# A third Q/K buffer, loads moved behind the row transfers, and half of the row transfers issued by ACT, in a fused token mixer

## The chip, the cores and the metric

One core of one Trainium2 chip runs the whole program. The metric is the device time of one execution in microseconds (us); lower is better. Time before: median 774.71 us of 3 runs.

## The reference, cut to what matters

The input has batch 4, 8 heads, 768 tokens and head size 48 (so 384 features). Three stages follow one another.

```python
# 1: recurrence per head, S complex [48, 48]; a = (a_re, a_im) scaled to |a| <= 0.999
for t in range(S):
    S_re, S_im = ar * S_re - ai * S_im + k_t v_t^T, ar * S_im + ai * S_re
    y[t] = q_t @ S_re
# 2: x from y, heads side by side: [4, 768, 384]
h = x.transpose(0, 2, 1) @ U @ V          # rank 32 over the tokens
u = x + h.transpose(0, 2, 1)
x = u + relu(u @ w_ch1) @ w_ch2           # 384 -> 1536 -> 384
# 3
theta = x @ w_theta
y = w_tok_r @ (x * cos(theta)) + w_tok_i @ (x * sin(theta))
u = x + y
out = u + relu(u @ w_ch)
```

## The kernel before

The recurrence is computed as chunked linear attention, six chunks of 128 tokens per batch element ("batch" below, b = 0 to 3; chunks c = 0 to 5). The complex decay is turned into real exponents and phases, so that Q and K of a chunk are multiplied by a decay factor and then by a cosine and by a sine of the phase. The cosine part is r = 0, the sine part is r = 1. Stages 2 and 3 are large fp32 matmuls. Each engine runs its own program, written out by hand, in which everything of one engine stands in a fixed order and all ordering between engines is by semaphores. There is no scheduler.

What happens for chunk c+2 and chunk c of the attention, with the names used below:

- SP issues the load of Q and K (`load_qk`, L330) into one of two buffers `qk_in`, which are parts of the big tile `stream`; 384 KB. The load of chunk c waits until chunk c-2 has been multiplied (`s_Q`).
- ACT computes the decay factors of chunk c+2 (`decays`, L682, six ACTIVATEs L691/L692) for b >= 1. For b = 0 they are ready before the loop.
- DVE multiplies Q and K in place by the factors (`scaled`, L1041) and then writes the cosine product and the sine product (`turned`, L1055), each of which raises `s_Q` by one.
- SP copies the two products into `rows` with a different layout, features of a head on the partitions (`to_rows`, L343). Each part is two DMAs, 256 KB (L357) and 128 KB (L358), so four DMAs per chunk. SP waits for `s_Q` before each part.
- PE transposes K of the product (`key_columns`, L1343), ACT copies that out (`keys_to_sbuf`, L710/L711, four ACTIVATEs), PE computes scores from `rows` (`scores`, 16 matmuls, 96x128), then keys times values (`keys_values`, 16 matmuls 128x96), then the outputs (`values`, 128x128 and 96x128), and transposes the state (`turn_state`, L1375).
- ACT copies keys times values (L735) and the chunk's output (L742, the output copy). DVE masks the scores (L1072) and updates the state (L1089, L1091).

ACT's order within a chunk c is: `keys_to_sbuf(c)`, `decays(c+2)`, `rows_of_x(c-1)` (L718), the copy L735, the output copy L742. In batch 0 two weight pieces are rounded after that (`round_piece`, L867). SP's order for c from 1 is: load of Q/K of chunk c+3, load of V of chunk c+2, rows of chunk c+2. `first_rows` (L651) already issues one pair of row DMAs from ACT, once, at the start of the program.

The two quoted lines that set the waits of a row transfer and of a Q/K load:

```python
sp.wait_ge(s_Q.sem, s_Q.at(b, c) + r + 1)      # L355, in front of each part
sp.wait_ge(s_Q.sem, s_Q.at(b, c - 1))          # L333, the load into a used buffer
```

Of the kernel before, what the change touches and what calls it, by code (L numbers as in the profile page):

```python
# [11 lines left out]
P = 128  # L12
# [17 lines left out]
def token_mixer_program(nc, v, qk_rows, a_rows, U, V, w1, w2, w_tc, w_tok, out):  # L30
# [18 lines left out]
    with ExitStack() as ctx:  # L49
# [42 lines left out]
        a_in = stream[:, 0:2 * A_BUFS * D].rearrange("p (i j d) -> p i j d", i=A_BUFS, j=2)  # L92
        qk_in = [stream[:, at * D:(at + 2) * D].rearrange("p (i j t) -> p i j t", i=G, j=2) for at in (0, 2)]
        tok = nc.alloc_sbuf_tensor_at("tok", [P, 4, 2, S], F32R, offset=stream_at)
# [119 lines left out]
        s_a_in = [sem(f"s_a_in{i}", 2 if i + A_BUFS < C else 1, 16) for i in range(A_BUFS)]  # L214
        s_qk_in = [sem(f"s_qk_in{i}", C // 2, 16) for i in range(2)]
        s_v_in = [sem(f"s_v_in{i}", C // 3, 16) for i in range(3)]
# [106 lines left out]
        def _(sp):  # L323
# [6 lines left out]
            def load_qk(b, c):  # L330

                if c >= 2:
                    sp.wait_ge(s_Q.sem, s_Q.at(b, c - 1))  # L333
                sp.dma_start(qk_in[c % 2], qk_rows[b, c * P:(c + 1) * P, :].rearrange("p (i j t) -> p i j t", i=G, j=2))\
                    .then_inc(s_qk_in[c % 2].sem, 16)

# [6 lines left out]
            def to_rows(b, c):  # L343

                if c >= 3:
                    sp.wait_ge(s_yt.sem, s_yt.at(b, c - 2))
                elif b and c == 2:
                    sp.wait_ge(s_ch.sem, s_ch.at(b - 1, 2 * KD))
                elif b and c == 1:
                    sp.wait_ge(s_mix.sem, s_mix.at(b - 1, 2 * C))  # L350
                elif b:
                    sp.wait_ge(s_mix.sem, s_mix.at(b - 1, 2 * C - 2))
                to = rows[c % 3]
                for r in range(2 if b or c else 1):
                    sp.wait_ge(s_Q.sem, s_Q.at(b, c) + r + 1)  # L355
                    wide, fine = row(r)
                    sp.dma_start(to[wide, :, :, :], QKz[c % 2][:, r, 0:2, :, :]).then_inc(s_rows_in[c % 3].sem, 16)  # L357
                    sp.dma_start(to[fine, :, :, :], QKz[c % 2][:, r, 2, :, :]).then_inc(s_rows_in[c % 3].sem, 16)  # L358
# [42 lines left out]
            def batch(b, last):  # L401
                b_next = b + 1
                for c in range(C - 1):
                    if c + 3 < C and (c >= 1 or b == 0):
                        load_qk(b, c + 3)
                    if c >= 1 and c + 2 < C:
                        load_v(b, c + 2)
                    if c + 2 < C:
                        to_rows(b, c + 2)
                    if b and c == 0:  # L410
                        sp.wait_ge(s_stored[2 * KD - 1].sem, s_stored[2 * KD - 1].at(b, 0))
                        load_v(b, 2)
                    if b and c == 1:
                        store(b - 1, KD)
                        store(b - 1, KD + 1)
# [9 lines left out]
                if not last:  # L425
                    load_a_last(b_next)
                    sp.wait_ge(s_tan.sem, s_tan.at(b_next, C))
                    sp.wait_ge(s_quot.sem, s_quot.at(b_next, C))
                load_tok(b, 0)
                load_tok(b, 1)  # L430
# [7 lines left out]
                if not last:  # L438
                    sp.wait_ge(s_mix.sem, s_mix.at(b, 2 * C - 3))
                    load_qk(b_next, 0)  # L440
                    load_qk(b_next, 1)
                    gains_to_rows(b_next)
                    to_rows(b_next, 0)
                    load_qk(b_next, 2)
                    sp.wait_ge(s_mix.sem, s_mix.at(b, 2 * C))
                    load_v(b_next, 0)
                    load_v(b_next, 1)
# [10 lines left out]
            for c in range(C):  # L458
                load_a(0, c)
            load_qk(0, 0)  # L460
            load_qk(0, 1)
            for i in range(3):
# [9 lines left out]
            to_rows(0, 0)  # L472
            load_qk(0, 2)
            to_rows(0, 1)
            gains_to_rows(0)
            for n in range(2 * PIECES, STAGED):
# [113 lines left out]
        def _(act):  # L590
# [51 lines left out]
            def first_sin_cos(c):  # L642
# [6 lines left out]
                a.activation(sin, sin, ACT.Sin, scale=SIN_TURN).then_inc(s_phasor.sem, 1)  # L649

            def first_rows():  # L651

# [69 lines left out]
            def attention(b, c):  # L722
# [17 lines left out]
                if c >= 1:  # L740
                    act.wait_ge(s_y.sem, s_y.at(b, c))
                a.activation(YT[:, :, :], heads(bank[3][:, :]), ACT.Copy).then_inc(s_yt_sb.sem, 1)  # L742

            def hidden(b, n):
# [144 lines left out]
        def _(dve):  # L889
# [144 lines left out]
            def scaled(b, c):  # L1034

                dve.wait_ge(s_qk_in[c % 2].sem, s_qk_in[c % 2].at(b, c // 2 + 1))
                dve.wait_ge(s_exp.sem, s_exp.at(b, c + 1))
                both, factor = qk_in[c % 2], scale[:, c % 2, :, :, :]
                if b == 0:
# [3 lines left out]
            def turned(b, c, r):  # L1043
# [9 lines left out]
                elif b:  # L1053
                    dve.wait_ge(s_mix.sem, s_mix.at(b - 1, 2 * C - 2))
                d.tensor_tensor(QKz[c % 2][:, r, :, :, :], qk_in[c % 2],  # L1055
                                by.unsqueeze(2).broadcast_to([P, G, 2, P]), ALU.mult).then_inc(s_Q.sem, 1)
# [611 lines left out]
```

## Time and profile before

| | |
|---|---|
| median of 3 runs | 774.71 us (773.43 to 777.81) |
| the profiled execution | 773.47 us |
| its span | 771.7 us |
| mean granted TensorE clock | 0.989 |
| busy: PE, DVE, ACT, POOL | 731.8 (95%), 499.9, 403.8, 223.6 us |
| DMA | 73.48 MB, mean 95 GB/s |
| attention of batch 0, 1, 2, 3 (us from the start) | 48 to 96, 237 to 275, 414 to 453, 592 to 630 |

The span is what the profiler recorded between the first and the last instruction of the program; the execution's own time is 1.8 us longer. Busy times are sums over one engine. In a timeline row the first number is the start and the second how long it lasted, both in us; "x16" is how many instructions it merges. A number in square brackets ("idle before") is the time in which the engine did nothing ahead of that instruction, with what ended it.

### The profile page before, as it was taken

What the parts mean: (1) busy time and instruction counts of PE and PEld (TensorE: products, weight loads), DVE (VectorE), ACT (ScalarE), POOL (GpSimd) and SP (SyncE); (2) the same over time, 40 slices, a digit from 0 to 9 for tenths busy, and PEclk for the clock granted to TensorE, in tenths of its full rate; (3) what the DMA queues carried; (4) which work ended last, traced back from release to release, by engine and by line L of the source; (5) the groups of instructions that cost most, each with busy time, mean ns of one, the idle gap of its engine ahead of it and who ended that gap; (6) DMA issues with size and microseconds to landing.
All of it is one profiled execution on the core that took longest, in us unless ns stands there. A gap on an engine that the chain in (4) does not pass through costs nothing.

```text
span 771.7 us, 13433 instructions
## 1 busy us (share of the span) xinstructions
PE 731.8 (95%) x5118; PEld 704.2 (91%) x5118; DVE 499.9 (65%) x905; ACT 403.8 (52%) x875; POOL 223.6 (29%) x175
## 2 busy tenths in 40 slices
PE   3588999999999999999999999999999999999998
PEld 3578799999999879999999879999999979999998
DVE  7759488798468657696558758597448832224534
ACT  7847456755365447664464537574464621223531
POOL 0006663533520063323430053232530010113350
PEclk9889999999999999999999999999999999999999
DMA  9566620100257750010246860010136940000121
GB/s 301 169 184 180 196 87 1 41 1 2 82 145 213 209 174 1 4 39 1 62 133 184 218 205 21 2 42 1 50 96 185 254 135 23 2 1 0 42 62 62
DMA packets 42735, 73.48 MB, mean 95 GB/s; under 512 B 8784, under 2 KB 23376, under 8 KB 42672
## 3 DMA queue, kind: packets, MB, share of 16 engines
q1 hardware_dynamic: 42384, 72.23, 31.9%
q8 instruction: 41, 0.67, 0.4%
q10 hardware_dynamic: 288, 0.39, 0.2%
q14 instruction: 22, 0.18, 0.1%
HBM read 48.96 MB, written 4.72 MB: 70 GB/s over the span
## 4 chain that ended last, share of the span: by engine, by line
PE 81%; DVE 7%; ACT 4%; DMA 4%; issue 2%; SPq 1%; DVEq 0%; ACTq 0%
PE bank L1302 78%; DMA stream<-stream 2%; DMA region<-stream 1%; PE bank L1507 1%; DVE stream L1041 1%; DVE logr L915 1%; DVE logr L911 1%; PE bank L1418 1%; PE bank L1343 1%; PE bank L1375 1%; SPq L357 1%; DVE phasor L904 1%; DVE stream L1055 0%; SPq L358 0%; DVE ST L1072 0%
## 5 line engine op out<-in xcount | busy, mean ns | idle before, releaser
L1302 PE MATMUL bank<-uT,w_sb 128*128 128x384 f32 x864 | 166.5, 339 | 0.0
L1302 PE MATMUL bank<-hT,w_sb 128*128 128x384 f32 x864 | 165.0, 336 | 0.0
L1302 PE MATMUL bank<-tok,z 128*128 128x384 f32 x864 | 158.7, 337 | 0.6 <-issue 0.2
L1302 PEld LDWEIGHTS bank<-uT,w_sb 128*128 128x128 f32 x864 | 151.6, 190 | 1.8 <-ACT uT L756 1.2
L1302 PEld LDWEIGHTS bank<-hT,w_sb 128*128 128x128 f32 x864 | 151.1, 188 | 0.3 <-DVE hT L1200 0.3
L1302 PEld LDWEIGHTS bank<-tok,z 128*128 128x128 f32 x864 | 149.3, 188 | 1.7 <-POOL tok L539 1.7
L1200 DVE SCALAR_TENSOR_TENSOR hT<-bank,hT 128x384 fp32r<-128x384 f32 x96 | 52.8, 550 | 68.1 <-ACT hT L748 67.7
L748 ACT ACTIVATE hT<-bank 128x384 fp32r<-128x384 f32 x96 | 46.4, 484 | 75.4 <-PE bank L1302 75.3
L539 POOL TENSOR_TENSOR tok<-tok_low,tok 128x768 fp32r<-128x768 f32 x20 | 38.2, 1909 | 86.7 <-ACT tok L778 86.7
L547 POOL TENSOR_TENSOR x_sb<-uT 128x384 f32<-128x384 f32 x24 | 25.1, 1077 | 104.1 <-DVE uT L1194 71.1
L514 POOL TENSOR_TENSOR logr<-stream 128x384 f32<-128x384 f32 x18 | 15.1, 841 | 102.1 <-DMA stream<-in_a 102.1
L534 POOL TENSOR_TENSOR w_sb<-w_raw,w_sb 128x768 fp32r<-128x768 f32 x12 | 26.1, 2189 | 63.7 <-ACT w_sb L867 63.7
L553 POOL TENSOR_TENSOR xs<-x_sb,xs 128x384 fp32r<-128x384 f32 x24 | 27.7, 1173 | 54.5 <-ACT xs L765 54.5
L1302 PE MATMUL bank<-tc_sb,xs 128*128 128x384 f32 x216 | 41.4, 335 | 0.0
L1072 DVE TENSOR_TENSOR ST<-bank,tri 128x512 f32<-128x512 f32 x48 | 32.5, 687 | 13.2 <-PE bank L1302 12.9
L1302 PE MATMUL bank<-xs,tc_sb 128*128 128x384 f32 x216 | 38.9, 337 | 0.0
L519 POOL TENSOR_TENSOR phasor<-stream,phasor 128x384 f32<-128x384 f32 x18 | 18.8, 1046 | 68.6 <-ACT phasor L665 68.6
L1302 PEld LDWEIGHTS bank<-tc_sb,xs 128*128 128x128 f32 x216 | 37.9, 188 | 0.0
L1302 PEld LDWEIGHTS bank<-xs,tc_sb 128*128 128x128 f32 x216 | 37.4, 188 | 0.0
L539 POOL TENSOR_TENSOR tok<-scale,tok 128x768 fp32r<-128x768 f32 x16 | 29.4, 1848 | 25.9 <-ACT tok L778 25.9
L1302 PE MATMUL bank<-region 96*128 96x128 f32 x256 | 33.3, 286 | 3.6 <-DMA region<-stream 3.6
L1302 PEld LDWEIGHTS bank<-region 96*128 96x128 f32 x256 | 31.7, 200 | 4.1 <-DMA region<-stream 4.0
(183 smaller groups left out, 1309.5 us busy)
## 6 DMA issues: line engine op xcount, KB each, us to landing
stream<-in_qk SPq DMA_DIRECT2D x24, 384.0 KB, 3.9
tok_low<-in_w_tok SPq DMA_DIRECT2D x20, 384.0 KB, 3.5
stream<-in_a SPq DMA_DIRECT2D x19, 384.0 KB, 3.8
scale<-in_w_tok SPq DMA_DIRECT2D x16, 384.0 KB, 4.2
w_raw<-in_w SPq DMA_DIRECT2D x12, 384.0 KB, 7.8
region<-qk SPq DMA_DIRECT2D x16, 256.0 KB, 3.6
region<-stream SPq DMA_DIRECT2D x15, 256.0 KB, 3.2
stream<-in_v SPq DMA_DIRECT2D x16, 192.0 KB, 4.3
```

The costliest lines, as they stand in the source:

```text
L357: sp.dma_start(to[wide, :, :, :], QKz[c % 2][:, r, 0:2, :, :]).then_inc(s_rows_in[c % 3].sem, 16)
L514: ins = g.tensor_tensor(to, part, part, ALU.mult)
L519: g.tensor_tensor(phasor[:, c, 1, :], a_part(b, c, 1), phasor[:, c, 1, :], ALU.mult)\
L534: g.tensor_tensor(part[1], raw, part[0].bitcast(F32), ALU.subtract).then_inc(s_split.sem, 1)
L539: g.tensor_tensor(tok[:, m % 4, 1, :], tok_raw(m)[1], tok[:, m % 4, 0, :].bitcast(F32), ALU.subtract)\
L547: g.tensor_tensor(x_sb[:, n, :], uT[:, 0, kd, :].bitcast(F32), uT[:, 1, kd, :].bitcast(F32), ALU.add)\
L553: g.tensor_tensor(xs[0][:, 1, n % KD, :], x_sb[:, n, :], xs[0][:, 0, n % KD, :].bitcast(F32), ALU.subtract)\
L748: a.activation(hT[:, n % 3, 0, :], hidden_bank[n % 3][:, 0:N2], ACT.Relu).then_inc(s_hid_hi.sem, 1)
L904: d.tensor_tensor(mag, mag, qk[:, c * D:(c + 1) * D], ALU.add).then_inc(s_den.sem, 1)
L1072: d.tensor_tensor(ST[:, 4 * i:4 * i + 4, :], heads(score_bank[i][:, :]), tri[:, :].unsqueeze(1).broadcast_to([P, 4, P]), ALU.mult)\
L1200: d.scalar_tensor_tensor(hT[:, n % 3, 1, :], hidden_bank[n % 3][:, 0:N2], 0.0, hT[:, n % 3, 0, :].bitcast(F32), ALU.max, ALU.subtract)\
L1302: return t.matmul(o, lhsT, rhs, start=start, stop=stop, is_transpose=turned)
```

## The change

A tile `qk_third` is added and Q/K loads go round over three buffers. The load of chunk c waits for chunk c-3. SP puts the rows of chunk c+2 in front of the Q/K load of chunk c+4 and of the V load of chunk c+2. The load of chunk 2 for the next batch goes to an earlier place, in front of the first token-weight load; in batch 0 it goes to the program's start. From the third chunk on SP issues only the cosine part of the rows. The sine part is issued by ACT (`sine_rows`), directly behind the output copy of chunk c, for chunk c+2.

```diff
-        qk_in = [stream[:, at * D:(at + 2) * D].rearrange("p (i j t) -> p i j t", i=G, j=2) for at in (0, 2)]
+        qk_third = sb("qk_third", [P, 2 * D])
+        qk_in = [at.rearrange("p (i j t) -> p i j t", i=G, j=2)
+                 for at in (stream[:, 0:2 * D], stream[:, 2 * D:4 * D], qk_third[:, :])]
...
-                if c >= 2:
-                    sp.wait_ge(s_Q.sem, s_Q.at(b, c - 1))
-                sp.dma_start(qk_in[c % 2], ...)
+                if c >= 3:
+                    sp.wait_ge(s_Q.sem, s_Q.at(b, c - 2))
+                sp.dma_start(qk_in[c % 3], ...)
...
-                for r in range(2 if b or c else 1):
+                for r in range(2 if c < 2 and (b or c) else 1):
...
                 for c in range(C - 1):
-                    if c + 3 < C and (c >= 1 or b == 0):
-                        load_qk(b, c + 3)
+                    if c + 2 < C:
+                        to_rows(b, c + 2)
+                    if c + 4 < C:
+                        load_qk(b, c + 4)
                     if c >= 1 and c + 2 < C:
                         load_v(b, c + 2)
-                    if c + 2 < C:
-                        to_rows(b, c + 2)
...
                     sp.wait_ge(s_quot.sem, s_quot.at(b_next, C))
+                    load_qk(b_next, 2)
                 load_tok(b, 0)
...
                     to_rows(b_next, 0)
-                    load_qk(b_next, 2)
...
-            load_qk(0, 0)
-            load_qk(0, 1)
+            for c in range(3):
+                load_qk(0, c)
...
             to_rows(0, 0)
-            load_qk(0, 2)
             to_rows(0, 1)
+            load_qk(0, 3)
             gains_to_rows(0)
...
+            def sine_rows(b, c):
+
+                if c >= 3:
+                    act.wait_ge(s_yt.sem, s_yt.at(b, c - 2))
+                elif b:
+                    act.wait_ge(s_ch.sem, s_ch.at(b - 1, 2 * KD))
+                act.wait_ge(s_Q.sem, s_Q.at(b, c + 1))
+                wide, fine = row(1)
+                act.dma_start(rows[c % 3][wide, :, :, :], QKz[c % 2][:, 1, 0:2, :, :]).then_inc(s_rows_in[c % 3].sem, 16)
+                act.dma_start(rows[c % 3][fine, :, :, :], QKz[c % 2][:, 1, 2, :, :]).then_inc(s_rows_in[c % 3].sem, 16)
...
                 a.activation(YT[:, :, :], heads(bank[3][:, :]), ACT.Copy).then_inc(s_yt_sb.sem, 1)
+                if c + 2 < C:
+                    sine_rows(b, c + 2)
...
-                both, factor = qk_in[c % 2], scale[:, c % 2, :, :, :]
+                both, factor = qk_in[c % 3], scale[:, c % 2, :, :, :]
```

ACT's program in a batch from the second on, at chunk 1, before. `region<-bank` L742 is the output copy, `qk<-bank` is `keys_to_sbuf`, `scale<-` are the decay factors, `x_sb<-bank` is `rows_of_x`, `tA<-bank` the copy of keys times values:

```order
L735 ACTIVATE tA<-bank 112x384 [waits s_kv_t,s_kv]
L742 ACTIVATE region<-bank 128x512 [waits s_y,s_yt]
L710 ACTIVATE qk<-bank 128x256 [waits s_kv,s_ktr]
L711 ACTIVATE qk<-bank 128x128
L710 ACTIVATE qk<-bank 128x256 [waits s_kv,s_ktr]
L711 ACTIVATE qk<-bank 128x128
L691 ACTIVATE scale<-logr,minus_mid 128x128 [waits s_qf,s_mid,s_logr]
L692 ACTIVATE scale<-logr,marks 128x128
```

The same place of ACT's program in the changed kernel:

```order
L748 ACTIVATE tA<-bank 112x384 [waits s_kv_t,s_kv]
L755 ACTIVATE region<-bank 128x512 [waits s_y,s_yt]
L661 DMA region<-qk 32x4x512 [waits s_Q,s_yt]
L662 DMA region<-qk 16x8x256
L723 ACTIVATE qk<-bank 128x256 [waits s_kv,s_ktr]
L724 ACTIVATE qk<-bank 128x128
L723 ACTIVATE qk<-bank 128x256 [waits s_kv,s_ktr]
L724 ACTIVATE qk<-bank 128x128
L704 ACTIVATE scale<-logr,minus_mid 128x128 [waits s_qf,s_mid,s_logr]
L705 ACTIVATE scale<-logr,marks 128x128
```

Two DMA issues with a wait for DVE's products now stand between the output copy and the copies of the keys and the decay factors.

SP's queue in the same batch before, from the load of Q/K of chunk 4 to the rows of chunk 4:

```order
L334 DMA stream<-in_qk 128x768 [waits s_Q]
L341 DMA stream<-in_v 128x384 [waits s_yt]
L357 DMA region<-qk 32x4x512 [waits s_Q,s_yt]
L358 DMA region<-qk 16x8x256
L357 DMA region<-qk 32x4x512 [waits s_Q]
L358 DMA region<-qk 16x8x256
L392 DMA out<-tB 128x384 [waits s_out]
L392 DMA out<-tC 128x384 [waits s_out]
L334 DMA stream<-in_qk 128x768 [waits s_Q]
L341 DMA stream<-in_v 128x384 [waits s_yt]
L357 DMA stream<-stream 32x4x512 [waits s_Q,s_yt]
```

And in the changed kernel, from the rows of chunk 3 to those of chunk 4:

```order
L359 DMA region<-qk 32x4x512 [waits s_Q,s_yt]
L360 DMA region<-qk 16x8x256
L336 DMA qk_third<-in_qk 128x768 [waits s_Q]
L343 DMA stream<-in_v 128x384 [waits s_yt]
L394 DMA out<-tB 128x384 [waits s_out]
L394 DMA out<-tC 128x384 [waits s_out]
L359 DMA stream<-stream 32x4x512 [waits s_Q,s_yt]
```

The sine pair is gone from SP, the cosine pair stands first, and the loads follow it.

## Rows read from the trace of the kernel before

**Rows 1.** The page, busy time of each engine (us, share, instructions).

```profile
PE 731.8 (95%) x5118; PEld 704.2 (91%) x5118; DVE 499.9 (65%) x905; ACT 403.8 (52%) x875; POOL 223.6 (29%) x175
```

**Rows 2.** Waits of PE: total us, times, longest.

```profile
PE bank L1302 <- DMA region<-stream: 3.6, 2, 3.3
PE bank L1302 <- DMA stream<-stream: 2.4, 3, 1.0
```

**Rows 3.** Timeline of PE, batch 1, keys times values of chunks 3 and 4: start, us.

```profile
256.23 0.87 PE L1302 MATMUL bank<-qk,stream 128*48 128x96 f32 x16
...
263.12 0.87 PE L1302 MATMUL bank<-qk,stream 128*48 128x96 f32 x16
```

**Rows 4.** Timeline of ACT, batch 1, chunks 1 and 2.

```profile
247.05 0.60 ACT L742 ACTIVATE region<-bank 128x512 f32<-128x512 f32 x1 [1.29 <-PE bank L1302]
247.90 0.52 ACT L710 ACTIVATE qk<-bank 128x256 f32<-128x256 f32 x1 [0.25 <-PE bank L1343]
...
248.83 0.40 ACT L711 ACTIVATE qk<-bank 128x128 f32<-128x128 f32 x1
...
250.45 0.41 ACT L692 ACTIVATE scale<-logr,marks 128x128 f32<-128x128 f32 x1
...
253.84 0.52 ACT L710 ACTIVATE qk<-bank 128x256 f32<-128x256 f32 x1 [0.25 <-PE bank L1343]
```

**Rows 5.** Timeline of DVE, batch 1: products of chunk 2, then of chunk 4.

```profile
241.03 1.83 DVE L1055 TENSOR_TENSOR stream<-stream,phasor 128x768 f32<-128x768 f32 x2
...
250.96 0.96 DVE L1041 TENSOR_TENSOR stream<-stream,scale 128x768 f32<-128x768 f32 x1 [0.26 <-ACT scale L692]
251.95 1.83 DVE L1055 TENSOR_TENSOR stream<-stream,phasor 128x768 f32<-128x768 f32 x2
```

**Rows 6.** Timeline of SP's queue, batch 1: rows of chunk 4, first and third DMA.

```profile
252.98 0.57 SPq L357 DMA_DIRECT2D stream<-stream  x1
...
254.24 0.60 SPq L357 DMA_DIRECT2D stream<-stream  x1
```

**Rows 7.** Timeline of ACT and its queue at the one row pair that ACT issues.

```profile
43.10 0.69 ACTq L655 DMA_DIRECT2D region<-stream  x1
...
43.83 0.61 ACTq L656 DMA_DIRECT2D region<-stream  x1
44.49 0.51 ACT L710 ACTIVATE qk<-bank 128x256 f32<-128x256 f32 x1 [0.36 <-issue]
```

**Rows 8.** Timeline of PE, keys times values of chunk 4, batches 2 and 3.

```profile
441.03 0.87 PE L1302 MATMUL bank<-qk,stream 128*48 128x96 f32 x16
...
617.99 0.87 PE L1302 MATMUL bank<-qk,stream 128*48 128x96 f32 x16
```

**Rows 9.** Timeline of DVE, products of chunk 2, batches 2 and 3.

```profile
417.96 1.83 DVE L1055 TENSOR_TENSOR stream<-stream,phasor 128x768 f32<-128x768 f32 x2
...
595.90 1.83 DVE L1055 TENSOR_TENSOR stream<-stream,phasor 128x768 f32<-128x768 f32 x2
```

**Rows 10.** Timeline of batch 0: products of chunk 2, rounding, values of chunks 3 and 4.

```profile
57.78 1.83 DVE L1055 TENSOR_TENSOR stream<-stream,phasor 128x768 f32<-128x768 f32 x2
...
59.25 1.57 ACT L867 ACTIVATE w_sb<-w_raw 128x768 fp32r<-128x768 f32 x2
...
76.85 0.43 PE L1302 MATMUL bank<-ST,stream 128*48 128x128 f32 x4 [0.81 <-DVE ST L1072]
...
83.92 0.43 PE L1302 MATMUL bank<-ST,stream 128*48 128x128 f32 x4 [0.78 <-DVE ST L1072]
```

**Rows 11.** DMA issues: queue, count, KB each, median us from issue to landing.

```profile
region<-stream SPq DMA_DIRECT2D x15, 128.0 KB, 3.4
...
region<-stream ACTq DMA_DIRECT2D x1, 128.0 KB, 4.7
```

**Rows 12.** Stretches: length, busy us of each engine, granted PE clock, DMA share, GB/s.

```profile
100.00:104.00 4.00, 4.00 (x17) 4.00 (x16) 2.74 (x5) 2.12 (x5) 4.00 (x5) 0.65 0.06 25
...
248.00:252.00 4.00, 4.00 (x57) 3.86 (x57) 3.32 (x6) 3.69 (x12) 0.00 (x0) 1.00 1.08 260
```

More of the change, by code:

```diff
@@ L214, in token_mixer_program @@
         s_a_in = [sem(f"s_a_in{i}", 2 if i + A_BUFS < C else 1, 16) for i in range(A_BUFS)]
-        s_qk_in = [sem(f"s_qk_in{i}", C // 2, 16) for i in range(2)]
+        s_qk_in = [sem(f"s_qk_in{i}", C // 3, 16) for i in range(3)]
         s_v_in = [sem(f"s_v_in{i}", C // 3, 16) for i in range(3)]
@@ L330, in load_qk @@
             def load_qk(b, c):
-                if c >= 2:
-                    sp.wait_ge(s_Q.sem, s_Q.at(b, c - 1))
-                sp.dma_start(qk_in[c % 2], qk_rows[b, c * P:(c + 1) * P, :].rearrange("p (i j t) -> p i j t", i=G, j=2))\
-                    .then_inc(s_qk_in[c % 2].sem, 16)
+                if c >= 3:
+                    sp.wait_ge(s_Q.sem, s_Q.at(b, c - 2))
+                sp.dma_start(qk_in[c % 3], qk_rows[b, c * P:(c + 1) * P, :].rearrange("p (i j t) -> p i j t", i=G, j=2))\
+                    .then_inc(s_qk_in[c % 3].sem, 16)
             def load_v(b, c):
@@ L1034, in scaled @@
             def scaled(b, c):
-                dve.wait_ge(s_qk_in[c % 2].sem, s_qk_in[c % 2].at(b, c // 2 + 1))
+                dve.wait_ge(s_qk_in[c % 3].sem, s_qk_in[c % 3].at(b, c // 3 + 1))
                 dve.wait_ge(s_exp.sem, s_exp.at(b, c + 1))
-                both, factor = qk_in[c % 2], scale[:, c % 2, :, :, :]
+                both, factor = qk_in[c % 3], scale[:, c % 2, :, :, :]
                 if b == 0:
@@ L1054, in turned @@
                     dve.wait_ge(s_mix.sem, s_mix.at(b - 1, 2 * C - 2))
-                d.tensor_tensor(QKz[c % 2][:, r, :, :, :], qk_in[c % 2],
+                d.tensor_tensor(QKz[c % 2][:, r, :, :, :], qk_in[c % 3],
                                 by.unsqueeze(2).broadcast_to([P, G, 2, P]), ALU.mult).then_inc(s_Q.sem, 1)
```

## The prediction, made before the changed kernel was run

> **What bounds the kernel now.** I read the page's busy times first. PE is busy 731.8 of 771.7 us [rows 1], so only about 40 us can be won anywhere, and anything that makes PE wait is paid in full. Second come PE's waits: transfers of rows end 3.6 and 2.4 us of them, five waits in all, of which one at the program's start is 3.3 us [rows 2]. So in the attention of batches 1 to 3 all waiting for rows is 2.7 us. Third, the timeline of one attention chunk on all engines, in batch 1. ACT starts its key copies at 247.90 and again at 253.84 [rows 4], so a chunk takes 5.94 us, which is PE's pace without a gap. Keys times values of chunk 3 start at 256.23 and those of chunk 4 at 263.12 [rows 3]: 6.89 us, so one of the waits for rows lies between them. DMA is busy all the time in this stretch (share 1.08 at 260 GB/s), with PE at full granted clock [rows 12]. This is a stage in which PE leads and ACT, DVE and DMA follow closely. What matters is how much slack ACT has, not how busy it is on average.
>
> **The third buffer and the new order on SP.** This takes the Q/K loads off the path: DVE may wait for them now, but PE pays for that only through the 2.7 us. Rows go first, so their landing should improve. The V load now stands behind the cosine pair and a Q/K load. It is issued for a chunk that PE reaches more than one chunk (5.94 us) later, so I cost that at nothing; if that cover went, keys times values would wait for V. The early load of chunk 2 goes where the engines' DMA is nearly idle: nothing. The most this part can give in batches 1 to 3 is 2.7 us.
>
> **The start.** Chunk 2's 384 KB no longer run beside the first rows. ACT's first pair landed after 4.7 us, where the same 128 KB from SP take 3.4 us in the median [rows 11]. PE waits for exactly that landing, so I take -1.2 us. Bounds: 0, and the whole 3.3 us of the wait [rows 2].
>
> **What an issue costs ACT.** SP takes 1.26 us for a pair (252.98 to 254.24 [rows 6]). ACT's one pair ran from 43.10, and the next ACTIVATE started at 44.49, with 0.36 us of idle time put down to issue [rows 7]. So the pair held ACT's program for 1.39 us. I take 1.30 us; bounds 1.26 and 1.39. The Trainium skill (DMA: Bandwidth & Descriptors, the section on the anatomy of one DMA) puts a sequencer's dispatch at some 50 ns, and calls descriptor generation small. By that, as an estimate, a pair would hold ACT for about 0.1 us; these rows show over ten times that, and the sum goes by them.
>
> **What it holds up.** Behind the output copy of chunk c, ACT now waits for the second product of chunk c+2, issues, and only then copies the keys of chunk c+1 and computes the decay factors of chunk c+3. DVE needs these factors for the products of chunk c+3, and ACT's next issue waits for those products. This closes a circle which did not exist while SP did the waiting. Its length from rows: `keys_to_sbuf` starts at 247.90 and the factors end at 250.86 (250.45 + 0.41) [rows 4]; DVE starts on them at 250.96 and its second product ends at 253.78 (251.95 + 1.83) [rows 5]. That is 5.88 us. With 0.07 us until the issue starts and 1.30 us of issue, one turn is 7.25 us, against PE's 5.94. So from the first wait on, ACT leads, and PE falls behind by about 1.3 us per chunk.
>
> Batches 1 to 3, in the times of the trace before. Batch 1: the second product of chunk 2 ends at 242.86 (241.03 + 1.83 [rows 5]). Three turns (21.75 us) lead to the issue for chunk 5, starting at 264.7. Then come 1.30 us of issue and 1.33 us of key copies (247.90 to 248.83 + 0.40 [rows 4]), and keys times values of chunk 4 start at 267.4. Before, they started at 263.12 [rows 3]: **+4.3 us**. That already contains the waiting for rows between chunks 3 and 4 that goes away. In all it is 24.5 us from the end of the product. Batch 2: 417.96 + 1.83 = 419.8 [rows 9], so 444.3 against 441.03 [rows 8]: **+3.3 us**. Batch 3: 597.7, so 622.2 against 617.99: **+4.2 us**. Sum +11.8. After chunk 4 nothing waits on ACT like this, and PE keeps the shift; the rows of chunk 5 have landed by then (issue ends at 266.0, 3.4 us to landing, scores of chunk 5 at about 270.4).
>
> Batch 0 has no decay factors in the loop, so no circle through DVE. But two weight pieces, 1.5 us, are rounded behind the output copy, and the second product of chunk 2 ends at 59.61 (57.78 + 1.83) [rows 10]; issue to 61.0, rounding to 62.5, key copies to 63.8. From then on the chain from key copies to key copies is: PE from keys times values to the output copy 2.7 us (chunk 2 in batch 1: 256.23 - 5.94 = 250.29 to 247.05 + 5.94 = 252.99 [rows 3, 4]), then issue 1.3, rounding 1.5, key copies 1.3: 6.9 us, near the pace of that stage, which is set by DVE's masks (76.85 to 83.92, 7.07 us [rows 10]). The issue also has to wait for DVE's product where that ends behind the output copy's start, and I take 7.3 us per chunk; bounds 6.9 and 7.6. Three chunks on, the keys of chunk 4 are there at 85.7, and values start 0.8 us later, at 86.5 instead of 83.92 [rows 10]: **+2.6 us**, between 1.4 and 3.5.
>
> **The sum.** +11.8 + 2.6 - 1.2 = +13.2 us on the profiled execution's 773.47 us, so 786.7 us. That execution lies 1.2 us under the median of the runs shown; on the median the same step gives **787.9 us**.
>
> A rule on the gain: the Trainium skill (same page, Issuing engines are not separate DMA queues) says that transfers from several issuing engines run on the same 16 DMA engines, and that only the issuing sequencer's time is saved. The profile agrees as far as it goes: DMA is full in this stretch [rows 12], so a second issuer could bring rows forward by one pair's issue at most, the 1.26 us above.
>
> **Rivals.**
> 1. *The issue hardly holds ACT, and the rows' waits go* (faster). If the pair took under 0.06 us of ACT's program, the circle would be 5.95 + 0.06, just about PE's period of 5.94, and nothing would be lost. PE then gains the 2.7 us and the start's 1.2: 773.47 - 3.9 = 769.6, or 770.8 on the median. It turns at this price: with every 0.1 us more, a batch loses 0.3. For it: only one issued pair exists in the trace, and it stands beside other work. Against it: the 0.36 us of idle time behind it [rows 7], and SP's 1.26 us. The Trainium skill's 50 ns would make this case. Chance 0.11.
> 2. *The circle does not add up*, by slack I did not see, and each batch pays only for its first late issue. In batch 1 that makes the keys of chunk 1 ready at 242.86 + 2.7 = 245.6, where PE wanted them at 256.23 - 2 x 5.94 = 244.35: 1.2 us late. 3 x 1.2, with 2 us for batch 0, less 1.2: +4.4, 779.1. Chance 0.13.
> 3. *It cancels*: half of that with all waits gone, within 0.5% of before (the smallest difference that a measurement of this kernel can tell), 774.7. Chance 0.04.
> 4. *PE's clock falls too.* The new gaps leave PE waiting 1.3 us in each chunk. After batch 0's attention, which had gaps of about 0.8 us in each chunk [rows 10], the granted clock was 0.65 between 100 and 104 [rows 12], that is, partly at 1.2 GHz instead of 2.4; batch 1 in its attention shows 1.00. One fall costs 4 x 0.35 = 1.4 us. Three falls add 4.2: 792. Chance 0.14, and the reason for the upper end.
> 5. *The circle as summed*: 787.9, chance 0.58.
>
> **How the numbers follow.** The issue's bounds move the sum by 9 turns and 3 last issues: from -0.5 to +1.1 us; issues that now and then take twice as long add up to some 3 us; the start's bounds are -2 and +1.2. The range 778 to 793.5 takes in the last case and nearly all of the fourth and second; left out are the first, the third and half of the rest at the edges. Slower by over 0.5%: cases 2, 4, 5 less a little, 0.84. Within: 0.05. Faster: 0.11.
>
> **What the changed profile would show.** ACT waits for DVE's product ahead of its DMA issues, and its key copies start about 1.35 us after the end of that product. PE has a new wait of about 1.3 us per chunk, ended by ACT's key copies, ahead of keys times values of chunks 1 to 4. PE's chunk period in batches 1 to 3 is near 7.2 us. DVE waits for the decay factors before L1041 and no longer for Q/K. Waits for rows in batches 1 to 3 are gone. If PE's period stays 5.94 us, the circle is wrong; if it is longer but ended by DVE or DMA, the place is wrong. A granted clock under 1 in the attention of batches 1 to 3, or in the 10 us after it, is case 4.

## The result, and the profile after

The changed kernel takes **796.27 us** (median of 4 runs, 794.26 to 797.25) against 774.07 us before: a ratio of 1.028, with a 95% interval of 1.026 to 1.030. It is slower, as forecast, but the loss is 22 us where 13 were forecast, and the time lies 2.8 us above the end of the range. The profiled execution took 797.25 us, its span is 795.5 us and its mean granted clock 0.974.

The page, busy times of the changed kernel:

```profile
PE 740.0 (93%) x5118; PEld 713.8 (90%) x5118; DVE 499.5 (63%) x905; ACT 401.6 (50%) x875; POOL 221.6 (28%) x175
```

PE executes the same instructions as before [rows 1], is 8 us longer at it, and idles some 16 us more. ACT's and DVE's busy times are nearly the same (2.2 and 0.4 us less): issuing DMAs is not counted, so the page's busy share of ACT shows nothing of what happened. The waits of PE in the changed kernel do:

```profile
PE bank L1317 <- issue: 23.1, 16, 2.4
PE bank L1317 <- DMA region<-stream: 2.8, 1, 2.8
```

The waits for rows in batches 1 to 3 [rows 2] are gone, and only the one at the start is left. In their place stand 16 new waits, four in each batch, 23.1 us in all. Their releaser is given as "issue", but the timeline of PE in batch 1 shows where they are (keys times values of chunks 1 to 4):

```profile
254.01 0.87 PE L1317 MATMUL bank<-qk,stream 128*48 128x96 f32 x16 [1.31 <-issue]
...
261.31 0.87 PE L1317 MATMUL bank<-qk,tD 128*48 128x96 f32 x16 [1.32 <-issue]
...
268.62 0.87 PE L1317 MATMUL bank<-qk,stream 128*48 128x96 f32 x16 [1.32 <-issue]
...
275.92 0.87 PE L1317 MATMUL bank<-qk,stream 128*48 128x96 f32 x16 [1.32 <-issue]
```

The chunks follow each other at 7.30 us instead of 5.94. The timeline of ACT in the same batch shows one turn, and that of DVE the part between:

```profile
256.68 0.60 ACT L755 ACTIVATE region<-bank 128x512 f32<-128x512 f32 x1 [0.40 <-PE bank L1317]
258.54 0.57 ACTq L661 DMA_DIRECT2D region<-qk  x1
259.14 0.67 ACTq L662 DMA_DIRECT2D region<-qk  x1
259.91 0.51 ACT L723 ACTIVATE qk<-bank 128x256 f32<-128x256 f32 x1 [2.63 <-issue]
...
262.45 0.39 ACT L705 ACTIVATE scale<-logr,marks 128x128 f32<-128x128 f32 x1
...
265.85 0.57 ACTq L661 DMA_DIRECT2D stream<-stream  x1
```

```profile
262.94 0.96 DVE L1056 TENSOR_TENSOR stream<-stream,scale 128x768 f32<-128x768 f32 x1 [2.24 <-ACT scale L705]
263.93 1.83 DVE L1070 TENSOR_TENSOR stream<-stream,phasor 128x768 f32<-128x768 f32 x2
```

The output copy is done at 257.28, but ACT's next ACTIVATE, the key copy, starts at 259.91: 1.26 us of waiting for DVE's second product and 1.37 us for the pair (258.54 to 259.91). The factors end at 262.84, DVE starts on them at 262.94, its product ends at 265.76, and the next pair starts at 265.85. From pair to pair that is 7.31 us. In the kernel before, ACT had idled 0.25 us ahead of the same key copy, for PE's transposes [rows 4], and DVE had idled 0.26 us for its factors [rows 5] where it now idles 2.24.

Comparing when the same instruction starts in the two profiled executions tells where the 23.8 us between them came from:

| instruction | before | after | shift |
|---|---|---|---|
| first scores, batch 0 | 48.57 | 49.36 | +0.8 |
| scores of chunk 5, batch 0 | 86.25 | 94.54 | +8.3 |
| keys times values, chunk 0, batch 1 | 239.33 | 247.61 | +8.3 |
| chunk 4, batch 1 | 263.12 | 275.92 | +12.8 |
| chunk 0, batch 2 | 416.26 | 429.07 | +12.8 |
| chunk 4, batch 2 | 441.03 | 457.58 | +16.6 |
| chunk 0, batch 3 | 594.20 | 611.93 | +17.7 |
| chunk 4, batch 3 | 617.99 | 640.23 | +22.2 |
| end of the span | 771.7 | 795.5 | +23.8 |

The attention of batches 1 to 3 costs 4.5, 3.7 and 4.5 us, together 12.8; batch 0's costs 7.5; 0.8 us come before it, and 1.2 and 1.6 us after the attention of batches 2 and 3. Batch 0 looks different. The timeline of ACT there, chunk 1, with the output copy's issue one and two turns later, then of DVE and POOL, and of PE:

```profile
67.39 0.60 ACT L755 ACTIVATE region<-bank 128x512 f32<-128x512 f32 x1 [1.28 <-PE bank L1317]
68.93 0.57 ACTq L661 DMA_DIRECT2D region<-qk  x1
69.52 0.68 ACTq L662 DMA_DIRECT2D region<-qk  x1
70.25 1.58 ACT L882 ACTIVATE w_sb<-w_raw 128x768 fp32r<-128x768 f32 x2 [2.26 <-issue]
71.73 0.50 ACT L723 ACTIVATE qk<-bank 128x256 f32<-128x256 f32 x1
...
77.42 0.60 ACT L755 ACTIVATE region<-bank 128x512 f32<-128x512 f32 x1 [0.95 <-PE bank L1317]
77.48 0.57 ACTq L661 DMA_DIRECT2D stream<-stream  x1
...
84.33 0.60 ACT L755 ACTIVATE region<-bank 128x512 f32<-128x512 f32 x1 [1.28 <-PE bank L1317]
85.77 0.57 ACTq L661 DMA_DIRECT2D region<-qk  x1
```

```profile
65.52 3.32 DVE L1070 TENSOR_TENSOR qk<-stream,phasor 128x768 f32<-128x768 f32 x2
...
71.99 4.95 DVE L1070 TENSOR_TENSOR stream<-stream,phasor 128x768 f32<-128x768 f32 x2
...
82.36 3.32 DVE L1070 TENSOR_TENSOR qk<-qk_third,phasor 128x768 f32<-128x768 f32 x2
```

```profile
62.85 4.31 POOL L536 TENSOR_TENSOR w_sb<-w_raw,w_sb 128x768 fp32r<-128x768 f32 x2 [60.46 <-ACT w_sb L882]
71.17 4.95 POOL L536 TENSOR_TENSOR w_sb<-w_raw,w_sb 128x768 fp32r<-128x768 f32 x2 [4.01 <-ACT w_sb L882]
79.68 4.32 POOL L536 TENSOR_TENSOR w_sb<-w_raw,w_sb 128x768 fp32r<-128x768 f32 x2 [3.56 <-ACT w_sb L882]
```

```profile
64.72 0.87 PE L1317 MATMUL bank<-qk,stream 128*48 128x96 f32 x16 [1.49 <-issue]
...
73.12 1.52 PE L1317 MATMUL bank<-qk,tD 128*48 128x96 f32 x16 [2.41 <-issue]
...
81.66 0.87 PE L1317 MATMUL bank<-qk,stream 128*48 128x96 f32 x16 [0.93 <-issue]
...
89.91 1.34 PE L1317 MATMUL bank<-qk,stream 128*48 128x96 f32 x16 [2.27 <-issue]
```

Three things are to be seen. An issue can follow the output copy's start in 0.06 us, as it does at 77.48; in chunk 1 it follows after 1.54 us (68.93), when DVE's product is done (65.52 + 3.32 = 68.84), and in chunk 3 after 1.44 us (85.77; the product ends at 85.68), with the rounding still behind it each time. The three pairs of products take 3.32, 4.95 and 3.32 us instead of 1.83 [rows 10], and all three start while POOL splits a weight piece; the longest ends at 76.94, before its output copy, so nothing waits for it. And after PE's gaps of 2.41 and 2.27 us, the same 16 matmuls take 1.52 and 1.34 us instead of 0.87. The stretches of the changed kernel from 72 and from 88 us say why (in each row, the granted clock is the third number from the end; the row from 20 us belongs to the start and is used further below):

```profile
20.00:24.00 4.00, 2.58 (x12) 2.58 (x12) 3.82 (x11) 3.97 (x10) 0.00 (x0) 0.50 0.87 219
72.00:76.00 4.00, 2.88 (x32) 2.90 (x33) 4.00 (x2) 2.65 (x7) 4.00 (x2) 0.63 0.65 198
88.00:92.00 4.00, 2.09 (x26) 2.11 (x28) 0.00 (x0) 2.62 (x7) 3.53 (x2) 0.77 0.54 115
```

PE's clock was at 1.2 GHz for part of the last two stretches. In the kernel before it was 1.00 all through the attention of batch 0 from 60 us on.

### The profile page after: what moved, and what is told of

Its sections match the earlier page's. It is cut to its first block, busy times and chain, and to the rows that moved or that the text cites. A ratio compares the mean times of both kernels' runs of the same rounds, so it can differ in the third digit from the quotient of the medians.

```text
span 795.5 us, 13448 instructions
## 1 busy us (share of the span) xinstructions
PE 740.0 (93%) x5118; PEld 713.8 (90%) x5118; DVE 499.5 (63%) x905; ACT 401.6 (50%) x875; POOL 221.6 (28%) x175
## 4 chain that ended last, share of the span: by engine, by line
PE 86%; DVE 5%; ACT 4%; issue 4%; DMA 1%; DVEq 0%; ACTq 0%
PE bank L1317 81%; PE bank L1358 2%; PE bank L1390 1%; PE bank L1433 1%; PE bank L1522 1%; DVE logr L930 1%; DVE logr L926 1%; DMA region<-stream 1%; DVE phasor L919 0%; ACT first_scale L634 0%; DVE hT L1215 0%; DVE Z L1196 0%; DMA stream<-in_a 0%; ACT phasor L675 0%; ACT qk L676 0%
## 5 line engine op out<-in xcount | busy, mean ns | idle before, releaser
L1317 PE MATMUL bank<-uT,w_sb 128*128 128x384 f32 x864 | 169.1, 343 | 0.0
L1317 PEld LDWEIGHTS bank<-uT,w_sb 128*128 128x128 f32 x864 | 154.7, 193 | 1.3 <-ACT uT L771 0.9
L723 ACT ACTIVATE qk<-bank 128x256 f32<-128x256 f32 x40 | 21.2, 529 | 50.3 <-issue 32.1
L536 POOL TENSOR_TENSOR w_sb<-w_raw,w_sb 128x768 fp32r<-128x768 f32 x12 | 24.5, 2059 | 72.0 <-ACT w_sb L882 72.0
```

The lines of the kernel that those rows point to most:

```text
L536: g.tensor_tensor(part[1], raw, part[0].bitcast(F32), ALU.subtract).then_inc(s_split.sem, 1)
L723: a.activation(Kn[:, :, to_wide].rearrange("p (h i) d -> p h i d", i=2), wide, ACT.Copy)
L1317: return t.matmul(o, lhsT, rhs, start=start, stop=stop, is_transpose=turned)
```

## The experiments

Nine kernels were run, and the change once more, each beside runs of the kernel before on the same chip. "Circle" is the closed chain: ACT issues, copies keys, computes factors; DVE makes the products; ACT's next issue waits for them.

### Only the third buffer and the new order

```diff
-                for r in range(2 if c < 2 and (b or c) else 1):
+                for r in range(2 if b or c else 1):
...
-                if c + 2 < C:
-                    sine_rows(b, c + 2)
```

> Third buffer and the new order on SP as in the change, but SP issues both parts of the rows, as before. Theory (ACT's issues behind the output copy cost the time): the waits for rows in batches 1 to 3 shrink or go and nothing is lost, 770.5 to 774 us, PE's chunk period in batch 1 is 5.94 us. Rival (the loads and V behind the rows are late, or the third buffer disturbs the start): most of the 22 us stays, above 785 us, and PE or DVE waits for Q/K or V loads.

Measured: 773.22 us against 774.34 (ratio 0.997, interval 0.995 to 0.9996). The loss is gone, and a small gain is left. PE's waits for DMA, in this kernel's list of waits:

```profile
PE bank L1315 <- DMA region<-stream: 2.8, 1, 2.8
PE bank L1315 <- DMA stream<-in_v: 0.2, 1, 0.2
```

Of the waits for rows only the start's is left; one of 0.2 us for a V load is new. In batch 1 keys times values of chunk 0 and chunk 4 start at 238.77 and 261.70, 22.93 us apart, against 23.79 before; over batches 1 to 3 this stretch is 3.0 us shorter in all. So this half of the change does what it says, and PE gets the little that the rows' waits held. Of those 2.7 us the time shows 1.1, with an interval from 0.3 to 3.7. The third buffer and the new order were not tried one without the other.

### Only the issues on ACT

The kernel before, with `sine_rows` and its call added and SP's loop cut to the cosine part from chunk 2 on:

```diff
-                for r in range(2 if b or c else 1):
+                for r in range(2 if c < 2 and (b or c) else 1):
...
+                if c + 2 < C:
+                    sine_rows(b, c + 2)
```

> The kernel before, with its two buffers and its order on SP, and only the sine part from the third chunk on issued by ACT. Theory: the whole loss is here, 793 to 798 us, with a chunk period of 7.3 us in batches 1 to 3. Rival (the new order on SP does most of it): under 780 us.

Measured: 797.03 us against 774.34 (ratio 1.029, interval 1.025 to 1.032), as slow as the whole change. Keys times values of this kernel in batch 1:

```profile
254.18 0.87 PE L1315 MATMUL bank<-qk,stream 128*48 128x96 f32 x16 [1.30 <-issue]
...
261.47 0.87 PE L1315 MATMUL bank<-qk,tD 128*48 128x96 f32 x16 [1.31 <-issue]
```

The turn is 7.29 us. The loss sits in the issues on ACT alone, and the rival that blamed the order of loads on SP is out. PE's waits for rows in batches 1 to 3 are gone here too, with two buffers and the old order: PE comes later. So their absence in the changed kernel says nothing for the third buffer; the first experiment does.

### ACT waits, but issues nothing

SP issues both parts, as in the first experiment; of `sine_rows` only the waits stay:

```diff
                 act.wait_ge(s_Q.sem, s_Q.at(b, c + 1))
-                wide, fine = row(1)
-                act.dma_start(rows[c % 3][wide, :, :, :], ...)
-                act.dma_start(rows[c % 3][fine, :, :, :], ...)
```

> The change, with ACT still waiting for DVE's second product behind its output copy, but issuing nothing; SP issues the sine part. Theory: the turn of the circle is then 7.3 less 1.35 us of issues, about 5.95 us, PE's own period, so 771 to 776 us and PE hardly waits for the key copies. Rival (the wait alone costs it, the issues are cheap): 788 us or more, with the period still above 7 us.

Measured: 774.86 us against 774.34 (ratio 1.001, interval 0.998 to 1.003). Key copies of this kernel in batch 1:

```profile
243.43 0.52 ACT L720 ACTIVATE qk<-bank 128x256 f32<-128x256 f32 x1 [1.23 <-DVE stream L1067]
...
249.38 0.52 ACT L720 ACTIVATE qk<-bank 128x256 f32<-128x256 f32 x1 [1.23 <-DVE qk L1067]
...
255.35 0.52 ACT L720 ACTIVATE qk<-bank 128x256 f32<-128x256 f32 x1 [1.24 <-DVE stream L1067]
```

ACT still waits 1.23 us for DVE in each chunk, but the turn is 5.95 us, which is PE's own. The wait closes the circle, and against the kernel before it costs nothing. Against the kernel of the first experiment, from which this one differs by the wait alone, it does cost a little: 774.86 to 773.22 us, 1.6 us (by the means 2.3, with a 95% interval from 0.9 to 3.6). In the traces, chunk 0 to chunk 4 of batches 1 to 3 are 1.1 us longer together, and batch 0 is 0.6 us longer. So the wait takes back what the first experiment had won, and it is the time of the issues that makes the circle longer than PE's chunk and costs the 22 us.

### Half the issues on ACT

ACT issues the 256 KB transfer of the sine part, SP the 128 KB one:

```diff
-                for r in range(2 if c < 2 and (b or c) else 1):
+                for r in range(2 if b or c else 1):
...
+                    if c < 2 or r == 0:
+                        sp.dma_start(to[wide, :, :, :], ...)
...
-                act.dma_start(rows[c % 3][fine, :, :, :], ...)
```

> The change with half the issues on ACT: ACT waits as in the change but issues only the 256 KB transfer; SP issues the 128 KB one of the sine part. Theory (the circle's turn is 5.95 us plus what ACT issues): a turn of 6.6 us, so batches 1 to 3 lose about 1.6, 0.8 and 1.6 us against the kernel before where the change loses 4.5, 3.7 and 4.5; batch 0 loses 2 to 3: 779 to 783 us. Rival (a second issuing queue or the wait costs it, not the number of issues): above 790 us.

Measured: 782.18 us against 774.37 (ratio 1.010, interval 1.006 to 1.014), as expected. Two key waits of PE in batch 1:

```profile
254.85 0.87 PE L1317 MATMUL bank<-qk,tD 128*48 128x96 f32 x16 [0.65 <-issue]
...
261.46 0.87 PE L1317 MATMUL bank<-qk,stream 128*48 128x96 f32 x16 [0.64 <-issue]
```

The turn is 6.61 us. With no, one and two issues it is 5.95, 6.61 and 7.31 us, and the times are 774.9, 782.2 and 796.3 us. In batches 1 to 3 the dose is straight. The times are not: two issues cost nearly three times what one does. In batch 0 the half-dose kernel needs 40.6 us from the first scores to those of chunk 5, where the kernel before needs 37.7 and the change 45.2, and its granted clock stays at 1.00 there from 60 us on, with gaps of 1.70 us at most. In batches 1 to 3 it loses 1.8, 0.8 and 1.8 us against the kernel before, where 1.6, 0.8 and 1.6 were expected.

### Batch 0 left to SP

```diff
-                for r in range(2 if c < 2 and (b or c) else 1):
+                for r in range(2 if (c < 2 or b == 0) and (b or c) else 1):
...
-                if c + 2 < C:
+                if b and c + 2 < C:
```

> The change, but in batch 0 SP issues the sine part; ACT does it in batches 1 to 3 alone. Theory: batch 0's attention gives back about 7.5 us and the circle in batches 1 to 3 stays (4.5, 3.7 and 4.5 us), so 787 to 790 us. Rival (batch 0's loss comes from the start, the extra Q/K load there or a clock that falls by chance): 792 us or more, and batch 0's chunk period stays above 8 us.

Measured: 784.77 us against 774.34 (ratio 1.014, interval 1.008 to 1.019), 2 us below what was expected. The circle in batches 1 to 3 stands (7.30 us in batch 1). Batch 0 gives back 11.5 us by the medians. By the traces, scores of chunk 5 are at 84.73 instead of 94.54, 9.8 us earlier, but 2.4 of these are there before the first issue on ACT: keys times values of chunk 0 start at 54.09 instead of 56.51. From there to the scores of chunk 5 it is 30.64 us here, 30.63 in the kernel before and 38.03 in the changed one. So the issues in batch 0 cost 7.4 us, as was expected; the rest of the 11.5 lies in the start and in executions that scatter from 781.1 to 789.4 us.

### The same issues, behind the key copies

```diff
                     keys_to_sbuf(b, c)
+                if 1 <= c < C - 1:
+                    sine_rows(b, c + 1)
...
-                if c + 2 < C:
-                    sine_rows(b, c + 2)
```

> The change with the same two issues on ACT, moved behind the next chunk's key copies and ahead of the decay factors. Theory (what counts is what is queued behind the wait): PE no longer waits for keys; the remaining circle (factors, products, issues) is about 6.15 us, and the sine part lands just about when the scores want it, so 775 to 782 us. Rival (ACT cannot carry 1.3 us more per chunk wherever it stands): above 789 us.

Measured: 777.66 us against 774.37 (ratio 1.006, interval 1.002 to 1.009). Moving the pair by four ACTIVATEs takes away 18.6 of the 22 us. What is left is only in part what was expected. This kernel's timeline of PE, in batch 1 and in batch 0:

```profile
257.73 2.05 PE L1317 MATMUL bank<-region 96*128 96x128 f32 x16 [1.12 <-DMA region<-qk]
```

```profile
79.10 0.43 PE L1317 MATMUL bank<-ST,stream 128*48 128x128 f32 x4 [2.62 <-DVE ST L1087]
```

The rows land late, but chunk 0 to chunk 4 of batches 1 to 3 are only 0.6 us longer in all than in the kernel before, which waits for rows as well (3.6 us longer than in the first experiment, which does not). Batch 0, from keys times values of chunk 0 to the scores of chunk 5, is 2.3 us longer (32.89 us). There one pair of products takes 3.47 us, PE waits 2.62 us for DVE's masks behind it, and the granted clock is 0.64 from 80 to 84 us. Either way, this placement is still worse than leaving the issues to SP.

### Batch 0 with the rounding first

```diff
                         round_piece(2 * c)
                         round_piece(2 * c + 1)
+                        if c + 2 < C:
+                            sine_rows(b, c + 2)
...
-                if c + 2 < C:
+                if b and c + 2 < C:
                     sine_rows(b, c + 2)
```

> The change, but in batch 0 ACT rounds its two weight pieces ahead of the wait and the issues instead of behind them. Theory (in batch 0 ACT sits idle waiting for DVE's product with the rounding behind it, and the long gaps lower PE's clock): the rounding fills that wait, the gaps of PE shrink from 2.3 us to under 1.5 us and the two falls of its clock there go, 788 to 792 us. Rival (ACT's load in batch 0 is what counts, not its order): 795 us or more, with the clock still falling between 72 and 96 us.

Measured: 787.10 us against 774.37 (ratio 1.016, interval 1.012 to 1.021), 0.9 us below what was expected. Timeline of ACT in batch 0, chunk 1:

```profile
63.30 0.83 ACT L884 ACTIVATE w_sb<-w_raw 128x768 fp32r<-128x768 f32 x1
63.72 0.57 ACTq L661 DMA_DIRECT2D region<-qk  x1
64.04 0.83 ACT L884 ACTIVATE w_sb<-w_raw 128x768 fp32r<-128x768 f32 x1
64.32 0.69 ACTq L662 DMA_DIRECT2D region<-qk  x1
65.11 0.53 ACT L723 ACTIVATE qk<-bank 128x256 f32<-128x256 f32 x1 [0.24 <-issue]
```

The sequencer issues the pair while the rounding, already handed over, still runs, and ACT is idle for 0.24 us instead of 2.26 (0.24 to 1.14 us over the four pairs). Keys times values of chunks 1 to 4 are at 60.14, 66.56, 73.72 and 80.18, 6.68 us apart on average, and the clock stays at 1.00 from 40 us to the end of the stage. All pairs of products take 1.83 us, and none of them starts while POOL splits a piece. From keys times values of chunk 0 to the scores of chunk 5 it is 30.80 us, against 38.03 in the changed kernel and 30.63 in the kernel before. Same work, same number of issues, and 7.2 of the 7.4 us are gone: in batch 0 it was the order on ACT. (By the medians it is 9.2 us; PE was 3.2 us less from the first scores to keys times values of chunk 0, before ACT's first issue, at a clock of 1.00 instead of 0.50 to 0.65.)

### Filler for PE in the two long gaps

```diff
-                for j in range(PAIRS):
-                    ins = t.transpose(heads(bank[5][:, :])[:, j, 0:112], ...)
+                for j in range(PAIRS * (4 if b == 0 and c in (1, 3) else 1)):
+                    ins = t.transpose(heads(bank[5][:, :])[:, j % PAIRS, 0:112], ...)
```

> The change, and PE repeats the four transposes of the output three more times (about 1.4 us of work that changes nothing) in batch 0, ahead of the keys times values of chunks 2 and 4, where it waits 2.4 and 2.3 us. Theory (these two gaps lower PE's clock and that costs 1.6 us each, on top of the gaps): the gaps shrink to about 1 us, the granted clock stays 1.00 between 60 and 98 us, and though PE does more work the time falls by 2 to 3.5 us against the change run beside it. Rival (the clock falls there whatever PE does, or its fall is covered): the same time or longer.

> The change unaltered, beside the kernel with the filler. Theory: 794 to 798 us, with PE's clock at 0.6 to 0.8 twice in batch 0's attention. Rival (the first result was a matter of the chip or the hour): outside of that.

Measured: 795.46 us with the filler, and 797.27 for the change beside it, both against 775.97. The second lies in the 794 to 798 us that were expected of it, with a granted clock of 0.76 from 72 us and 0.68 from 92 us, so the first result was not a matter of the chip. From the first scores to those of chunk 5 the profiled executions take 43.4 us with the filler and 45.4 without. Stretches of the kernel with the filler:

```profile
72.00:76.00 4.00, 1.94 (x35) 1.76 (x35) 3.96 (x3) 3.32 (x8) 3.23 (x2) 1.00 0.83 210
88.00:92.00 4.00, 2.83 (x47) 2.65 (x47) 0.47 (x1) 3.16 (x8) 3.50 (x2) 1.00 0.63 143
```

With more work for PE, the gaps are 2.06 and 1.17 us (about 1 was expected of both), the clock does not fall, and the stage is 2.0 us shorter. That is what the two falls cost, less what the filler itself takes. The medians differ by 1.8 us, slightly less than the 2 to 3.5 expected, and no more than the spread of the runs. The ranges of the two overlap (792.97 to 796.35 and 794.36 to 799.26), so the shown part is the trace.

### The load at the start

The kernel of the first experiment, with batch 0's load of chunk 2 back between the first two row transfers.

```diff
-            for c in range(3):
+            for c in range(2):
                 load_qk(0, c)
...
             to_rows(0, 0)
+            load_qk(0, 2)
             to_rows(0, 1)
```

> Third buffer and new order, SP issues everything, and the load of chunk 2 of batch 0 is back between the first two row transfers. Theory that this load delayed the first sine rows (my -1.2 us): the wait of PE for the first rows is 3.3 us again where it is 2.8 without it, and the time is 0.5 to 1.2 us above the kernel in which only SP issues. Rival (the start is set by something else, such as the clock): the same time within 0.5 us.

Measured: 773.28 us against 774.37, where the first experiment had 773.22 against 774.34 (intervals 0.997 to 1.001 and 0.995 to 0.9996): no difference in the time, as the rival had it. PE's wait for the first rows is 3.23 us with the load there and 2.77 us without it, so the load costs 0.5 us of waiting at that place, as the theory had it, and the time does not show it.

## Why the prediction was right, and where it was wrong

**Direction and mechanism: right.** The new waits are ahead of keys times values of chunks 1 to 4; their cause, shown by taking the issues away while leaving the wait, is the circle. No rival's mechanism took its place; the fourth rival's sign, a clock under 1 just behind the attention, did show twice and is taken up below.

**The price of a pair: right.** 1.30 us were taken between 1.26 and 1.39; the trace has 1.37 in the turn shown, and 1.32 to 1.59 over the twelve pairs of batches 1 to 3. The turn was summed to 7.25 us and is 7.31.

**Batches 1 to 3: nearly right.** Forecast 4.3, 3.3 and 4.2 us, measured 4.5, 3.7 and 4.5.

**Batch 0: the step that failed.** I wrote "I take 7.3 us per chunk; bounds 6.9 and 7.6". It is 8.4 us (64.72, 73.12, 81.66, 89.91), and values of chunk 4, for which the +2.6 us were worked out, start at 90.98 instead of 83.92. From the first scores to those of chunk 5 batch 0 loses 7.5 us, far over the upper bound of 3.5.

Taken apart by the same rows, the three turns are 8.40, 8.54 and 8.25 us. The pair, the rounding and the key copies are as summed. Two pieces are not. The wait for DVE's product is 1.54, 0.06 and 1.44 us, where 7.3 leaves 0.4 for it. And in the second turn PE takes 4.30 us from keys times values to the output copy, instead of 2.67 in the two others, because its clock had fallen.

Behind the first piece stands a length that I took from chunk 2's products, 1.83 us. Here the products overlap POOL's splitting of the weights, which starts when ACT has rounded a piece, so it moves when ACT's order moves. In the kernel before it lay beside other DVE instructions, and there these were the long ones:

```profile
60.25 3.98 POOL L534 TENSOR_TENSOR w_sb<-w_raw,w_sb 128x768 fp32r<-128x768 f32 x2 [57.86 <-ACT w_sb L867]
```

```profile
62.60 2.45 DVE L1041 TENSOR_TENSOR stream<-stream,first_scale 128x768 f32<-128x768 f32 x1
65.09 1.83 DVE L1055 TENSOR_TENSOR qk<-stream,phasor 128x768 f32<-128x768 f32 x2
```

(0.95 us is the same scaling for chunk 2, clear of POOL.) The kernel that rounds first shows that the order was the cost. That POOL is what lengthens DVE's instructions is read from the coincidence in these traces and was not tried by itself.

The second piece is the clock. I put its fall (rival 4) behind the attention of batches 1 to 3, for gaps of 1.3 us. It also came inside batch 0, behind gaps of 2.41 and 2.27 us, a size that I had not forecast. The filler shows 2.0 us of net cost.

**The start: wrong.** "-1.2 us" took the whole difference between ACT's landing and SP's median as the load's doing. The load was worth 0.5 us (3.2 to 2.8 us of wait). The first scores came 0.8 us later, not 1.2 earlier: ACT issued its first pair 1.26 us later (44.36 instead of 43.10 [rows 7]). Up to 21 us the two traces are alike in DVE's times to 0.1 us, but PE's granted clock between 20 and 24 us is 0.89 before and 0.50 after. In the profiled executions of the experiments the first scores start between 46.9 and 50.7 us, and the changed kernel itself has 49.36 once and 50.14 the other time. So the start differs from one execution to the next by as much as the change makes there.

**After the attention of batches 2 and 3,** 1.2 and 1.6 us of the difference between the two traces are single falls of the clock, in these stretches:

```profile
472.00:476.00 4.00, 3.81 (x13) 3.60 (x13) 3.59 (x7) 1.36 (x3) 2.70 (x3) 0.57 0.58 216
656.00:660.00 4.00, 4.00 (x15) 3.91 (x16) 1.50 (x3) 0.76 (x2) 2.87 (x3) 0.59 0.75 290
```

This is the sign that the prediction had named for rival 4. But the kernel in which SP issues all has such falls too (0.76 and 0.82 in the stretches from 452 to 460 us, 0.63 from 632), without any new gap, and the half-dose kernel has none. So I do not count them to the change. What decides where they come stays open.

**The range.** The case "clock falls too" carried the upper end, at 792 plus a little, on top of a batch 0 term with 0.9 us of room. Batch 0 and the start together were 6.9 us off, and that is what put the result beyond it. With 1.0 us more in batches 1 to 3 and the 2.8 us of the two falls, that is the 10.6 us between the 786.7 us forecast for the profiled execution and its 797.25.

**The third buffer** with the new order gives what its term said: the waits for rows in batches 1 to 3 are gone, and the time gains 0.3 to 3.7 us where 2.7 was the most that was forecast. With the issues left to SP this is the fastest version tried, by a median of 1.1 us in both kernels that have it; only in the first of them is the gain clear of the noise. "I cost that at nothing", of V, is 0.2 us off in the first experiment's trace.

## What to carry to other kernels

Before a DMA issue goes to an engine that computes, follow what is queued behind its wait until the chain returns to the same engine. If it closes, the sum of its pieces is the new period, and it costs little (here 1.6 us) until it passes the leading engine's own. An issue waits best behind whatever others need from that engine: here four ACTIVATEs of difference in place were worth 18.6 of 22 us, and rounding ahead of the issues 7.2 of the 7.4 us of batch 0. To compare stages of two executions, start the clock at the first instruction that the change can reach, not at the stage's first. Each stage with other neighbours (here batch 0, with POOL at work and rounding on ACT) needs its own chain with its own durations.

## What the runs showed of the hardware that I had not expected

A pair of DMA issues of 256 and 128 KB holds ACT's program for 1.32 to 1.59 us in batches 1 to 3, and shows in no busy time. The Trainium skill (DMA: Bandwidth & Descriptors, the anatomy of one DMA) has some 50 ns for a sequencer's dispatch, in a section on DMAs that GpSimd issues; each of the issues here, which ACT makes, occupied its queue for 0.57 to 0.85 us. The estimate of 0.1 us for a pair, in the prediction, carried that figure over to ACT, and the trace does not bear it out. But ACTIVATEs that were handed over before it go on running: with the rounding in front, the same pair left ACT idle for only 0.24 us.

PE's clock fell after single gaps of 2.41 and 2.27 us in batch 0, and again in the two other profiled executions that have these gaps (2.42 and 2.32 us; 2.44 and 2.28 us in the kernel with only the issues on ACT). It did not fall during the chunks with gaps of 1.3 us each (batches 1 to 3), with gaps of 1.7 us (half the issues), or after one gap of 2.06 us (the filler). The length of a gap alone does not settle it: in the kernel that rounds first PE waited 2.76 us for its first rows, and its clock was 1.00 from 40 us to the end of batch 0's attention. Repeating 12 transposes that change nothing, in each of two places, kept it up in batch 0, and made the stage 2.0 us shorter.
